# Attention and two feed-forward blocks on one core: input loads of the attention part issued by ScalarE instead of SyncE

## The reference

```python
# q, k, v: (4, 8, 576, 64); x: (2304, 512) after the heads are joined
q_rot, k_rot = rotate(q), rotate(k)              # rotary embedding, halves of 32
scores = (q_rot @ k_rot.T) / 8
attn = exp(scores - max(scores)); attn /= (sum(attn) + 1e-9)
x = (attn @ v) as (B*S, H*D)
h = x @ w_in;  x = (h - tanh(h)) @ w_out         # 512 -> 2048 -> 512
h = x @ moe2_w_in; out = (h * sigmoid(h)) @ moe2_w_out
```

## Time and profile before

| | |
|---|---|
| three runs, median | 1149.1 us (1148.83 to 1150.8) |
| the profiled execution's own time | 1147.84 us |
| its span in the trace | 1146.1 us |
| attention part | 0 to about 337 us |
| feed-forward part | about 337 to 1146 us |
| DMA queues in use by the kernel | one, 55.68 MB |

### The profile page before, as it was taken

The page is one execution under the profiler, slowest core; times in us unless marked ns, Lnnn a source line. Parts: engine busy times, 40 slices in busy tenths (PEclk is TensorE's granted clock), DMA queues, the critical chain, the costliest instruction groups (busy, mean ns, idle before and its releaser), DMA issues.

```text
span 1146.1 us, 16702 instructions
## 1 busy us (share of the span) xinstructions
PE 1085.8 (95%) x6672; PEld 996.2 (87%) x6672; DVE 454.1 (40%) x728; ACT 433.1 (38%) x783; POOL 288.1 (25%) x123
## 2 busy tenths in 40 slices
PE   2788999889999999999999999999999999999998
PEld 1667777778789999999999999989999989999897
DVE  4466666666635232323223234442323222232322
ACT  1456676676762232323223232322323232232322
POOL 6647877777356000000000003730000000000000
PEclk9899999999999999999999999999999999999999
DMA  4432434343115100000000002300000000000000
GB/s 134 164 125 86 135 124 141 118 142 99 42 40 186 38 1 1 1 0 0 0 0 0 0 0 73 111 36 1 28 0 27 0 27 0 0 27 0 28 0 27
DMA packets 39691, 56.25 MB, mean 49 GB/s; under 512 B 21088, under 2 KB 21344, under 8 KB 37728
## 3 DMA queue, kind: packets, MB, share of 16 engines
q1 hardware_dynamic: 39648, 55.68, 15.1%
HBM read 46.27 MB, written 4.79 MB: 45 GB/s over the span
## 4 chain that ended last, share of the span: by engine, by line
PE 78%; POOL 7%; DMA 4%; DVE 4%; SPq 2%; issue 2%; ACT 2%; ACTq 0%; POOLq 0%; DVEq 0%
PE ps L592 34%; PE ps L611 17%; PE ps L606 17%; PE ps L528 4%; PE ps L496 2%; POOL raw L371 2%; DMA R<-inverse_sums 1%; DVE pl L786 1%; DVE hm L775 1%; PE ps L463 1%; DMA raw<-qk 1%; POOL wout_l L396 1%; POOL raw L365 1%; POOL win_l L396 1%; POOL xT L388 1%
## 5 line engine op out<-in xcount | busy, mean ns | idle before, releaser
L592 PE MATMUL ps<-xs_h,win_l 128*128 128x384 f32 x768 | 258.5, 337 | 3.0 <-POOL xs_l L430 1.7
L592 PE MATMUL ps<-xs_h,win_h 128*128 128x384 f32 x768 | 257.6, 335 | 0.0
L592 PE MATMUL ps<-xs_l,win_h 128*128 128x384 f32 x768 | 257.2, 335 | 0.0
L740 ACT ACTIVATE g_h<-ps 128x384 fp32r<-128x384 f32 x192 | 94.5, 492 | 300.1 <-PE ps L611 134.8
L734 ACT ACTIVATE act<-ps 128x384 f32<-128x384 f32 x192 | 94.5, 492 | 255.2 <-PE ps L592 255.2
L592 PEld LDWEIGHTS ps<-xs_h,win_l 128*128 128x128 f32 x768 | 144.2, 188 | 9.3 <-issue 3.9
L592 PEld LDWEIGHTS ps<-xs_l,win_h 128*128 128x128 f32 x768 | 144.2, 188 | 3.4
L592 PEld LDWEIGHTS ps<-xs_h,win_h 128*128 128x128 f32 x768 | 144.1, 188 | 0.0
L775 DVE TENSOR_REDUCE hm<-ps 128x2 f32<-128x576 f32 x144 | 108.7, 757 | 60.8 <-PE ps L463 60.1
L606 PE MATMUL ps<-g_h,wout_h 128*128 128x384 f32 x384 | 128.3, 334 | 0.0
L606 PE MATMUL ps<-g_h,wout_l 128*128 128x384 f32 x384 | 128.3, 334 | 0.0
(11 more groups left out here) (73 smaller groups left out, 1554.5 us busy)
## 6 DMA issues: line engine op xcount, KB each, us to landing
raw<-qk SPq DMA_DIRECT2D x15, 1152.0 KB, 6.2
w_stage<-w_in SPq DMA_DIRECT2D x8, 1024.0 KB, 5.2
w_stage<-w_out SPq DMA_DIRECT2D x8, 1024.0 KB, 5.6
R<-inverse_sums SPq DMA_DIRECT2D x32, 144.0 KB, 3.1
vr<-vin SPq DMA_DIRECT2D x16, 256.0 KB, 3.7
out<-ostage SPq DMA_DIRECT2D x5, 768.0 KB, 3.6
ev<-ev SPq DMA_DIRECT2D x16, 144.0 KB, 2.3
hl<-hl SPq DMA_DIRECT2D x30, 64.0 KB, 2.2
```

The source lines that it names most:

```text
L592: last = mm(o, w[g][:, kk, c:c + 128], x[:, kk, :], start=(n == 0), stop=(n == 11))
L740: nc.scalar.activation(g_h[f % 2][:, :], ps[:, 4 + f % 4, 0:TN], ACT.Copy, scale=(1.0, 0.5)[L]).then_inc(s_gh, 1)
```

## The change

The three functions that load q and k, the split values and the unsplit values move from SyncE's program to ScalarE's, unchanged but for the engine that waits and issues. At the start ScalarE issues, ahead of all its work, q and k of pair 1 and the values of pairs 0 and 1 (6 transfers); `load(2)` comes behind its `copy_rows(0)`. In pair n it issues `load_split_v(n + 1)` and `load(n + 3)` ahead of the exponentials of step k = 0, and `load_full_v(n + 1)` ahead of those of step k = 2. SyncE keeps the tables, q and k of pair 0, the identity, and all the other transfers.

```diff
             for i in range(2):
                 sp.dma_start(raw[0][:, i:4:2, :], qk[0, :, i:4:2, :]).then_inc(s_ld0[i], 16)
-            sp.dma_start(raw[1][:, :, :], qk[1, :, :, :]).then_inc(s_ld[1], 16)
             sp.dma_start(idf[:, :], ident).then_inc(s_id, 16)
-            load_split_v(0)
-            load_full_v(0)
-            load_full_v(1)
...
             sp.wait_ge(s_lq, 1)
             copy_blocks(0, slice(QL, KL + 1, 2), s_bd[0])
-            load(2)
             sp.wait_ge(s_lq, 2)
...
             for n in range(PAIRS):
-                if n + 1 < PAIRS:
-                    load_split_v(n + 1)
-                if n + 3 < PAIRS:
-                    load(n + 3)
                 if n >= 1:
                     gather_sums(n - 1)
                     join_heads(n - 1)
-                    if n + 1 < PAIRS:
-                        load_full_v(n + 1)
...
+            def load(n):
+                sc.wait_ge(s_lq, n - 1)
+                sc.dma_start(raw[n % 2][:, :, :], qk[n, :, :, :]).then_inc(s_ld[n % 2], 16)
+
+            def load_split_v(n):
+                if due(n):
+                    sc.wait_ge(s_vl, n)
+                sc.dma_start(vr[:, :, :, :], vin[n, :, 1:5, :, :]).then_inc(s_vr, 16)
+
+            def load_full_v(n):
+                if n >= 2:
+                    sc.wait_ge(s_pv, 10 * (n - 1))
+                for h in range(2):
+                    sc.dma_start(quarters(v1[n % 2])[:, :, 3 * h, :], vin[n, :, 0:1, h, :]).then_inc(s_vf[n % 2], 16)
...
+            load(1)
+            load_split_v(0)
+            load_full_v(0)
+            load_full_v(1)
             qk_high(0)
             v_high(0)
             qk_high(1)
             sc.wait_ge(s_tm, 1)
             copy_rows(0, XB)
+            load(2)
             for n in range(PAIRS):
                 for k, units in enumerate(STEPS):
+                    if k == 0 and n + 1 < PAIRS:
+                        load_split_v(n + 1)
+                    if k == 0 and n + 3 < PAIRS:
+                        load(n + 3)
                     if k == 1:
                         move_out(n - 1, 1)
+                    if k == 2 and 1 <= n < PAIRS - 1:
+                        load_full_v(n + 1)
```

More of the change, by code:

```diff
@@ L237, in _ @@
                     w_src.append(w_out[512 * g:512 * g + 512, :].rearrange("(f p) d -> p f d", p=128))
[L239 to L252, removed]
             def copy_blocks(n, slots, done):
```

## The result

The changed kernel takes 1182.43 us (median of 4 runs, 1180.31 to 1184.32) against 1149.72 (4 runs): the ratio is 1.0284, 95% interval 1.0262 to 1.0305. The prediction was 1153.9, range 1146 to 1161. The sign was right, the size wrong by a factor of seven. The two profiled executions, 1184.32 and 1147.84 us, lie further apart than the medians: 36.5 us and not 32.7.

The account below looks back on a forecast made before the run. It took PE to bound the kernel, with R's loop nearly as long. Terms 2.6 - 1.5 + 2.6 + 1.2 + 2.2 - 2.3 = +4.8 us on 1147.84 gave 1152.6, as a median 1153.9, range 1146 to 1161.

Parts of the forecast that it names:

- What bounds it: PE and R's loop through ACT, SP and POOL are nearly equal, 0.15 to 0.3 us slack; nothing moves after 337 us.
- The head of a pair, R: Spread inverse R shares the engines with loads issued earlier on ACT: 0.4 us a pair, +2.6 us in all.
- The maxima: Heads of pairs 1 to 3: loads move ahead onto max_rows, whose landing PE awaits; 0.4 us each, +1.2 us.
- The start: Pair 1's loads, issued beside pair 0's, delay DVE's first operation and all behind it: +2.6 us, bounds 0 to 3.3.
- load(2): Pair 2's q and k, issued by ACT 2.1 us sooner, shorten waits of POOL and PE: -1.5 us.
- The third step: Two load_full_v issues on ACT between qk_high and the next exponentials: 0.28 us in 8 pairs, +2.2 us.
- The second rival: ACT issues a transfer only when its engine has finished, delaying third-step exponentials: +17.6 us, 1166.7 us; chance 0.10.
- What SP gains: With fewer issues, SP is no longer late with max_rows and sums in pairs 6 and 9: -2.3 us.
- The first rival: A separate queue helps SP's small transfers behind q and k, and load(2): -3.0 us, 1146.1 us; chance 0.24.

Follow-up runs that it names:

- the run with one queue: Kernel before, all transfers on SyncE, q and k of pair n + 4 moved ahead of R's two issues: 1180.02 us, ratio 1.0275.
- e1_full_v: Kernel before, with only the unsplit values of pairs 2 to 15 issued by ScalarE in the third step: 1148.84 us, ratio 0.9995.
- e13_all_step1: Kernel before, the loop's loads on ScalarE, with q, k and split values ahead of step k = 1; start and load(2) unchanged: 1146.57 us, ratio 0.9983.
- the kernel that beats both: Kernel before, the loop's loads on ScalarE, q, k and split values ahead of step k = 1, load(2) on ScalarE too: 1145.62 us, ratio 0.9949.

## Why the prediction was wrong, step by step

**What bounds it** was right: the feed-forward part didn't move, the two loops of a pair are that close, and what is added to R's loop comes out of PE.

**The head of a pair, R: the term that failed.** I took 0.4 us a pair, upper bound 0.8. Measured: R took 7.7 us and not 3.9 in the pair shown. Two things were wrong in it. The place: I had the issue behind the dispatch of the last exponential, 0.5 us ahead of it (134.1 for 134.57); the trace has the values' issue 1.1 us ahead (129.25 for 130.36), since the last exponential that had to wait was the one at 128.71, three before it. So R's second issue and q and k's fall together. The size: I let R share bandwidth, with the 256 KB of values in front of it. What stands in front of its second half is the values and the 1152 KB of q and k as well (3.0 us at 393 GB/s, 3.7 with the values; measured 3.8). The upper bound should have been all of the bytes issued ahead, as in one queue; the run with one queue gives much the same loss (1.0275), with R held up in more pairs (97.0 us of waits against 92.6) and the maxima not at all.

**The maxima**: 0.4 us a pair, upper bound 0.6 from a transfer beside other company. Measured in pair 3: 6.82 us to landing and not 2.27, PE idle for 5.54 us and not 0.99. In all 13.0 us of PE's waits against 3.5 in the kernel before. The same mistake: the bound was a row that had no such load beside it. From 104.0 to 107.1 us the profile has 205 packets on ACT's queue and none on SP's; 225 of SP's follow by 109.0, and 15 by 112.0. The bytes in front explain the first of these delays; what held the last packets back is not shown.

**The clock** had no term. A wait of 3 us on PE cost 3 us and then 3.4 or 6.8 us at half clock, by the estimate above some 0.9 us more work for each 3.4; most of the 8.8 us of longer work is that. In the trace of before PE's idle times from pair 4 on are at most 1.2 us and there is no such stretch there, so I had not thought of it (there are two earlier, below); the term belongs to every step that makes PE wait for longer.

**The start**: 2.6 us for DVE's first operation. Measured: 9.97 and not 7.73, 2.24 us.

```profile
9.97 0.76 DVE L814 TENSOR_TENSOR raw<-raw,ctab 128x576 f32<-128x576 f32 x1 [6.22 <-DMA raw<-qk]
```

**load(2)** was issued 26.18 - 14.46 = 11.7 us behind POOL's first operation, as forecast. The two terms together were +1.1, measured 0.0 (-1.8 to +1.8, the run with the start alone); load(2) alone gave -2.3 by its ratio (-4.0 to -0.6) where -1.5 stood.

**The third step**: 0.28 us a pair, 2.2 in all. Measured: 0. The issues did begin with `qk_high` (141.01) and not while it waited, as the trace of before showed for the semaphore instructions, but they take 0.82 us on ACT and not 1.07, and the next exponential came 1.07 us after `qk_high` as before (142.07 - 141.00). The second rival, 17.6 us for it, is out by the same rows. (Its bound of 1.24 us a pair should have been 1.21, 1.17 + 1.11 - 1.07; the 17 us were reckoned with 1.2.)

**What SP gains**: SP was late no more (16 of 16 calls of `max_rows` waited for ACT's copy), but the -2.3 us for it are not in the time of e1_full_v (-0.6, with an interval of -2.3 to +1.1 us), where q and k stay on SP. With all three kinds moved and out of R's way (e13_all_step1) the kernel gains 2.0 us (0.0 to 3.9), so a gain of about that size is neither shown nor out.

```profile
SPq L252 <- ACT rows L645: 38.5, 16, 9.0
```

The first rival had the sign wrong for the loop. But its load(2) is real, and it is part of the kernel that beats both.

## What to carry to other kernels

A big load that nobody waits for soon still has a place in time: a small transfer on the path that was issued right behind it (1152 KB, 3 us at 393 GB/s) came late by up to all of that, from the same queue or from another. Bound such a term by all the bytes issued ahead, and order loads by what else is in flight, not by which sequencer has time. The issues themselves were free on ScalarE, where it paused or had a long operation running.

## What the runs showed of the hardware

- A second queue didn't let small transfers by. Behind 256 and 1152 KB on ACT's queue, transfers of at most 2 KB on SP's queue took 6.82 us to land and not 2.27. The second half of R, issued 0.15 us or more behind the load of q and k, had no packet moved from 132.7 to 134.2 us, while 68 of the load's moved. With pieces of 2304 B and not 9216 B in the load the kernel's loss was the same (1.0303 and 1.0284).
  The Trainium skill, "DMA: Bandwidth & Descriptors", section "Queues, rings and completion order", has each DMA engine take turns between its queues, a packet at a time, with typically about 9 to 17 descriptors in a packet and at most 64. An estimate from that figure, if a piece is one descriptor: the load's 128 pieces of 9216 B are 8 to each of the 16 engines, so a packet can hold an engine's whole share, and a small transfer then waits for all of it; the trace agrees. With pieces of 2304 B there are 32 to an engine, and typical packets would let R in sooner. The trace of that run does not agree, unless the packets were larger: from 132.6 to 134.0 us 203 packets of the load moved, and 1 of SP's queue. Its section "Issuing engines are not separate DMA queues" says that transfers of all issuers share the same 16 engines and that a second issuer saves sequencer time alone; that agrees, with 1.0275 from one queue and 1.0256 from two.
- ACT issued the values in less time than SP: the unsplit ones in 0.45 us for SP's 0.585 (medians), the split ones in 0.353 for 0.584. q and k took 0.444 us for 0.430.
- ACT's sequencer issued transfers while ACT worked, but in the two places shown not while an operation ahead waited for a semaphore: the issues at 129.25 and 141.01 began 0.54 and 0.01 us behind the start of the operation that had waited (128.71 and 141.00).
- With each of PE's 8 idle times of 3.0 us or more from pair 1 on, its granted clock fell to 0.50 for 3.4 or 6.8 us, 37.4 us in all. It fell between 2.2 us before PE's next matmul and 1.7 us behind it. In the attention part of the kernel before it was at 0.50 for 10.2 us: 6.8 us with an idle time of 2.88 us (it fell at 42.3, PE began at 43.08), and 3.4 us from 107.1 on, where no idle time in the 10 us before was longer than 1.0 us. An idle time of 2.19 us there (until 57.58) had no such stretch. So the length of one idle time alone doesn't tell it. The start is not in these sums: the view gives 1.00 for it, but the same matmuls took longer than later (two of line 472 in 0.44 us at 42.07 and in 0.29 at 47.07), so there too the clock must have been low.
